# Delta-rule attention, ELU network and routed experts on one core: state products on four array quarters, a second output bank, norm steps and rounding pieces at other places

## The reference, cut to what matters

```python
# attention: 4 batches x 8 heads, 768 tokens, head size 48
k_n = k / (norm(k) + 1e-6)
for t in range(768):
    y[t] = q[t] @ state
    state += beta[t] * outer(k_n[t], v[t] - state.T @ k_n[t])
# then, on 3072 tokens of 384 features
x = elu(y @ w_in) @ w_out            # hidden 2048
logits = x @ w_gate + log1p(exp(x @ w_noise)) * noise
out = sum over the top 2 of 8 experts: weight * (relu(x @ w1[e]) @ w2[e])   # hidden 1024
```

## Time and profile before

| | us |
|---|---|
| median of three timed runs | 1183.45 (1182.54 to 1184.74) |
| the profiled execution's own time | 1186.29 |
| span of its instructions | 1184.5 |
| PE busy, share of the span | 1133.6 (96%) |
| DVE busy | 648.5 (55%) |
| ACT busy | 461.3 (39%) |
| POOL busy | 356.1 (30%) |
| mean granted TensorE clock | 0.991 |

### The profile page before, as it was taken

One profiled execution on the slowest core, in us unless ns is written; L12 is line 12 of the kernel. 1 busy time (PEld: TensorE's weight loads), 2 busy tenths in 40 slices (PEclk: granted clock), 3 DMA queues, 4 the chain that ended last, 5 costly groups with the idle time before them and its releaser, 6 DMA issues.

```text
span 1184.5 us, 29112 instructions
## 1 busy us (share of the span) xinstructions
PE 1133.6 (96%) x11596; PEld 1078.9 (91%) x11596; DVE 648.5 (55%) x1552; ACT 461.3 (39%) x1048; POOL 356.1 (30%) x378
## 2 busy tenths in 40 slices
PE   5897999898999999999999999999999999999996
PEld 3895788676999999999999999999999999999995
DVE  5888777763446556564655657522535353434442
ACT  1235556666333333333343335422424243333331
POOL 4289796244000120211202012322222222223223
PEclk9999999999999999999999999999999999999998
DMA  7453445853999110101101011472424242424221
GB/s 156 130 126 72 110 102 141 216 153 99 391 363 325 62 42 20 41 34 47 41 20 41 1 63 57 172 230 65 170 64 170 64 172 74 171 87 158 64 72 52
DMA packets 82603, 137.30 MB, mean 116 GB/s; under 512 B 11050, under 2 KB 70034, under 8 KB 81466
## 3 DMA queue, kind: packets, MB, share of 16 engines
q1 hardware_dynamic: 68490, 87.97, 25.8%
q0 software_dynamic: 12992, 28.75, 7.6%
q10 hardware_dynamic: 1008, 18.97, 4.3%
HBM read 81.96 MB, written 53.77 MB: 115 GB/s over the span
## 4 chain that ended last, share of the span: by engine, by line
PE 73%; DVE 1%; issue 0%; ACT 0%; POOL 0%; ACTq 0%; POOLq 0%
PE ps_x L1385 18%; PE ps_x L1475 18%; PE ps_h L1374 17%; PE ps_h L1453 17%; PE ps_r L1433 2%; PE ps_r L1424 1%; DVE hg L1793 0%; ACT hg L1583 0%; POOL out_dram L1340 0%; DVE w_parts L1756 0%; PE ps_r L1492 0%; DVE x_raw L1786 0%; PE ps_r L1402 0%; ACT yT_d L1601 0%; PE ps_r L1400 0%
## 5 line engine op out<-in xcount | busy, mean ns | idle before, releaser
L1475 PE MATMUL ps_x<-hg,w_parts 128*128 128x400 f32 x1152 | 230.2, 346 | 0.0
L1385 PE MATMUL ps_x<-w_parts,hg 128*128 128x400 f32 x1152 | 229.6, 345 | 0.0
L1374 PE MATMUL ps_h<-xg,w_parts 128*128 128x384 f32 x1152 | 222.3, 338 | 0.0
L1453 PE MATMUL ps_h<-xg,w_parts 128*128 128x400 f32 x1116 | 220.6, 345 | 1.1 <-DVE w_parts L1756 1.1
L1385 PEld LDWEIGHTS ps_x<-w_parts,hg 128*128 128x128 f32 x1152 | 209.7, 188 | 0.0
L1374 PEld LDWEIGHTS ps_h<-xg,w_parts 128*128 128x128 f32 x1152 | 204.0, 188 | 2.5 <-DVE elu_parts L1650 2.5
L1453 PEld LDWEIGHTS ps_h<-xg,w_parts 128*128 128x128 f32 x1116 | 202.7, 188 | 4.0 <-issue 3.1
L1475 PEld LDWEIGHTS ps_x<-hg,w_parts 128*128 128x128 f32 x1152 | 206.0, 188 | 0.0
L1793 DVE SCALAR_TENSOR_TENSOR hg<-ps_h,hg 128x400 fp32r<-128x400 f32 x128 | 73.5, 574 | 241.4 <-ACT hg L1583 238.6
L1320 POOL DMA_INDIRECT xs_scratch<-x,rows_now x48 | 49.3, 1027 | 393.5 <-DVE rows_now L1730 294.6
L1583 ACT ACTIVATE hg<-ps_h 128x400 fp32r<-128x400 f32 x128 | 64.7, 505 | 254.5 <-PE ps_h L1453 250.2
(11 more groups left out here) (175 smaller groups left out, 1325.9 us busy)
## 6 DMA issues: line engine op xcount, KB each, us to landing
xs_scratch<-pads SPq DMA_DIRECT2D x2, 5502.0 KB, 41.9
x_rows<-xs_scratch SPq DMA_DIRECT2D x17, 614.1 KB
kqT<-in_kqT_dram SPq DMA_DIRECT2D x48, 192.0 KB, 4.3
carried<-in_w_dram ACTq DMA_DIRECT2D x3, 3072.0 KB
w_raw<-in_w_dram ACTq DMA_DIRECT2D x3, 3072.0 KB
xs_scratch<-pads SPq DMA_DIRECT2D x6, 1375.5 KB, 16.8
out_dram<-pads SPq DMA_DIRECT2D x1, 4800.0 KB, 29.3
xs_scratch<-pads SPq DMA_DIRECT2D x6, 786.0 KB
```

Source lines behind the costliest of these rows:

```text
L1374: mm = nc.tensor.matmul(ps_h[f % 2][:, 0:TB], wi[:, a, k, f * P:(f + 1) * P], xr[:, b, k, :], start=(i == 0), stop=(i == len(passes) - 1))
L1385: mm = nc.tensor.matmul(ps_x[t][:, 0:DG], act_r[:, f % RING, a, t * P:(t + 1) * P], wo[:, b, f, :], start=(f == 0 and i == 0), stop=(f == ...
L1453: mm = nc.tensor.matmul(ps_h[f % 2][:, 0:TR], w1, xg[:, b, k, :], start=(m == 0), stop=(m == len(passes) - 1))
L1475: mm = nc.tensor.matmul(ps_y[k][:, 0:TR], w2r[i][:, a, s, k * P:(k + 1) * P], hg[:, s % RING, b, :], start=(s == 0 and m == 0), stop=(s == ...
```

## The change

- `ps_y` becomes two banks (4 and 5). The output of pair of heads p and half h goes to bank p % 2 and to rows `64 * (h ^ p % 2)`. The state's products contract over 48 rows (a half) in place of 128, four of them together, before the chunk's own four.
- The updates of the state, of both parities, move to bank 1, beside the keys on the state of odd chunks; `updates` gets one more wait.
- The outputs of a chunk are stored by four DMAs of half the size in place of two; the counts waited for double.
- `KEEP_BUSY` goes from 12 to 29.
- DVE: `to_set_lanes(2,(4,))` moves from ahead of the loop to the end of pair 0, (5,) and the squares to the end of pair 1; the other norm steps of group 2 move from the middle of pair 1 to pair 2, three single steps between its other work and four (`gains`) at its end. `place(1,0)` moves from the end of pair 2 into pair 3, `place(2,1)` from inside pair 7 to its end.
- ACT: the three rounding pieces of a pair move forward, to before `take_solved(a,1)`, `take_solved(b,1)` and `take_solved(a,2)`; `root_of(2)` moves to pair 2.

```diff
-KEEP_BUSY = 12
+KEEP_BUSY = 29
-        ps_y, ps_s = psum[:, 4], psum[:, 5]
+        ps_y = psum[:, 4:6, 0:2 * P].rearrange("p b (q t) -> p b q t", t=P)
+        ps_s = [psum[:, 1, i * NP * DH:(i + 1) * NP * DH] for i in range(2)]
+        def output_rows(p, h):
+            return slice(PADH * (h ^ p % 2), PADH * (h ^ p % 2) + DH)
             def store(n):
-                for h in range(2):
-                    sp.dma_start(xt_dram.rearrange("(p h d) t -> h d p t", h=2, d=DH)[h, :, :, at:at + C], yT[n % 2][heads(h)]
-                                 ).then_inc(outputs_stored[n % 2], 16)
+                for b in range(2):
+                    for h in range(2):
+                        sp.dma_start(xt_dram.rearrange("(q e d) t -> e d q t", e=4, d=DH)[2 * b + h, :, :, at:at + C],
+                                     yT[n % 2][output_rows(b, h)].rearrange("d (q b) t -> d q b t", b=2)[:, :, b]
+                                     ).then_inc(outputs_stored[n % 2], 16)
 # outputs, on PE
-                for p in range(NP):
-                    for h in range(2 if n >= B else 0):
-                        nc.tensor.matmul(ps_y[heads(h), p * P:(p + 1) * P], state[n % B][:, p, h * DH:(h + 1) * DH],
-                                         kqT[n % DEEP][:, p // QP, 1, p % QP, :], start=True, stop=False)
-                    for h in range(2):
-                        mm = nc.tensor.matmul(ps_y[heads(h), p * P:(p + 1) * P], x[n % KEPT][:, 2 * p + h, :],
+                for q in range(NP // 2):
+                    four = [(p, h) for p in (2 * q, 2 * q + 1) for h in range(2)]
+                    for p, h in four if n >= B else ():
+                        nc.tensor.matmul(ps_y[output_rows(p, h), p % 2, q], state[n % B][heads(h), p, h * DH:(h + 1) * DH],
+                                         kqT[n % DEEP][heads(h), p // QP, 1, p % QP, :], start=True, stop=False)
+                    for p, h in four:
+                        mm = nc.tensor.matmul(ps_y[output_rows(p, h), p % 2, q], x[n % KEPT][:, 2 * p + h, :],
                                               lq[n % KEPT][:, 2 * p + h, 1, :], start=(n < B), stop=True)
 # updates, on PE
+                if n >= 2:
+                    pe.wait_ge(rhs_ready[1], n // 2)
 # ACT, pair m
+                if m == 2:
+                    root_of(2)
                 if now:
+                    round_next()
                     take_solved(a, 1)
+                    round_next()
                     take_solved(b, 1)
                     round_next()
                     take_solved(a, 2)
...
-                    if m == 1:
-                        root_of(2)
-                    round_next()
                     take_solved(b, 2)
...
                     take_solved(a, 3)
-                    round_next()
 # DVE, pair m
-            to_set_lanes(2, (4,))
...
                 residuals(a, 1)
+                if m == 2:
+                    invert_root(2)
...
+                if m == 2:
+                    divide_by_root(2)
+                if m == 3:
+                    place(1, 0)
                 residuals(a, 2)
+                if m == 2:
+                    refine_root(2)
...
-                if m == 1:
-                    take_norms(2)
-                    turn_norms(2)
-                if m == 7:
-                    place(2, 1)
...
-                if m == 0:
-                    to_set_lanes(2, (5,))
+                if m < 2:
+                    to_set_lanes(2, (4 + m,))
+                if m == 1:
                     square_norms(2)
                 if m == 2:
-                    place(1, 0)
+                    gains(2)
+                    turn_norms(2)
...
-                if m == 6:
-                    place(2, 0)
+                if m in (6, 7):
+                    place(2, m - 6)
```

More of the change, by code:

```diff
@@ L364, in _ @@
                 if m == PAIRS - 2:
-                    sp.wait_ge(outputs_stored[0], (2 * B // 2 + 1) * 32)
+                    sp.wait_ge(outputs_stored[0], (2 * B // 2 + 1) * 64)
                     sp.wait_ge(vn_ready, NIT)
@@ L584, in updates @@
                         u = 2 * p + h
-                        mm = nc.tensor.matmul(ps_s[heads(h), at + p * DH:at + (p + 1) * DH], k_in[n % K_DEEP][:, u, :],
+                        mm = nc.tensor.matmul(ps_s[n % 2][heads(h), p * DH:(p + 1) * DH], k_in[n % K_DEEP][:, u, :],
                                               x[n % KEPT][:, u, :], start=True, stop=True)
@@ L710, in take_outputs @@
                 if n >= 2:
-                    act.wait_ge(outputs_stored[n % 2], n // 2 * 32)
-                nc.scalar.activation(yT[n % 2][0:PADH + DH], ps_y[0:PADH + DH].rearrange("p (a t) -> p a t", t=P), ACT.Copy
+                    act.wait_ge(outputs_stored[n % 2], n // 2 * 64)
+                nc.scalar.activation(yT[n % 2][0:PADH + DH].rearrange("p (q b) t -> p b q t", b=2), ps_y[0:PADH + DH], ACT.Copy
                                      ).then_inc(yT_ready, 1)
@@ L756, in _ @@
                     root_of(0)
-                take_blocks(i)
                 if i == 8:
                     root_of(1)
+                take_blocks(i)
                 for f in chunks_with(i):
@@ L838, in square_norms, with after_step @@
                                         ).then_inc(norm_step, 1)
[L840 to L852, removed]
-                dve.wait_ge(rooted, g + 1)
[L854 to L858, removed]
+            def after_step(g, k):
+                dve.wait_ge(norm_step, g * NORM_STEPS + k)
+                return slice(g * GSETS, (g + 1) * GSETS)
@@ new lines, in invert_root, with divide_by_root, refine_root @@
+            def invert_root(g):
+                sets = after_step(g, 1)
+                dve.wait_ge(rooted, g + 1)
+                nc.vector.reciprocal(root_inv[:, sets], root[:, sets]).then_inc(norm_step, 1)
+            def divide_by_root(g):
+                sets = after_step(g, 2)
+                nc.vector.tensor_tensor(quot[:, sets], norm2[:, sets], root_inv[:, sets], ALU.mult).then_inc(norm_step, 1)
+            def refine_root(g):
+                sets = after_step(g, 3)
+                nc.vector.tensor_tensor(root[:, sets], root[:, sets], quot[:, sets], ALU.add).then_inc(norm_step, 1)
@@ L859, in take_norms, with gains @@
+            def gains(g):
+                sets = after_step(g, 4)
+                nc.vector.tensor_scalar(norm_lane[:, sets], root[:, sets], 0.5, EPS, ALU.mult, ALU.add).then_inc(norm_step, 1)
+                after_step(g, 5)
+                nc.vector.reciprocal(root_inv[:, sets], norm_lane[:, sets]).then_inc(norm_step, 1)
                 if g == 0:
                     dve.wait_ge(beta_loaded, 16)
-                step(nc.vector.tensor_tensor(gain[:, sets], beta_sb[:, sets], root_inv[:, sets], ALU.mult))
@@ L862, in take_norms @@
-                step(nc.vector.tensor_tensor(gain[:, sets], gain[:, sets], root_inv[:, sets], ALU.mult))
+                after_step(g, 6)
+                nc.vector.tensor_tensor(gain[:, sets], beta_sb[:, sets], root_inv[:, sets], ALU.mult).then_inc(norm_step, 1)
+                after_step(g, 7)
+                nc.vector.tensor_tensor(gain[:, sets], gain[:, sets], root_inv[:, sets], ALU.mult).then_inc(norm_step, 1)
+                after_step(g, 8)
+            def take_norms(g):
+                invert_root(g)
+                divide_by_root(g)
+                refine_root(g)
+                gains(g)
@@ L915, in update_state @@
                     dve.wait_ge(ks_done[n % 2], (n - B) // 2 + 1)
-                at = n % 2 * NP * DH
                 for h in range(2):
                     s = state[n % B][heads(h), :, h * DH:(h + 1) * DH]
-                    nc.vector.tensor_tensor(s, s, ps_s[heads(h), at:at + NP * DH].rearrange("p (a d) -> p a d", d=DH), ALU.add
+                    nc.vector.tensor_tensor(s, s, ps_s[n % 2][heads(h)].rearrange("p (a d) -> p a d", d=DH), ALU.add
                                             ).then_inc(state_updated[n % 2], 1)
@@ L947, in _ @@
             dve.wait_ge(from_lanes, GSETS)
-            nc.vector.memset(ps_y, 0.0).then_inc(y_cleared, 1)
-            to_set_lanes(2, (4,))
+            nc.vector.memset(psum[:, 4:6], 0.0).then_inc(y_cleared, 1)
             for m in range(PAIRS):
@@ L1239, in _ @@
             for i in range(2):
-                sp.wait_ge(outputs_stored[i], PAIRS * 32)
+                sp.wait_ge(outputs_stored[i], PAIRS * 64)
             sp.dma_start(x_raw[:], xt_v[:, :, TB:2 * TB]).then_inc(x_loaded, 16)
@@ L1294, in _ @@
             for i in range(2):
-                pool.wait_ge(outputs_stored[i], PAIRS * 32)
+                pool.wait_ge(outputs_stored[i], PAIRS * 64)
             nc.gpsimd.memset(ones[:], 1.0).then_inc(consts_set, 1)
```

1 line of the change is left out of this document (removed).

## The result

| | before | after |
|---|---|---|
| median of the comparison, us | 1185.66 (1182.54 to 1189.29) | 1188.97 (1185.55 to 1194.5) |
| span of the profiled execution, us | 1184.5 | 1187.2 |
| mean granted clock | 0.991 | 0.991 |

The ratio is 1.003, 95% interval 1.0019 to 1.0041: slower by 3.3 us. The second part starts at 297.2 us of the span, 2.7 later than in the earlier trace rows, and takes as long as before. So, as in the prediction, everything is decided in the twelve pairs.

The account below looks back on a forecast made before the run. PE runs unbroken from 294.54 us, so only that start can move; pairs 3 to 6 are PE-bound. +2.7 (end of pair 8) - 2.1 (pairs 9 and 10) = +0.6, from the median 1183.45 giving 1184.0 us, range 1177.5 to 1189.5.

Parts of the forecast that it names:

- third rival: SP becomes the bound and the clock falls at each wait for keys in pairs 4 to 7: 1188.3 us, chance 0.16.
- Start: Loop start: first ACT copy 4.26 us earlier with fewer keep-clock matmuls, +1.8 for a cold clock in pair 0.
- Pairs 1 and 2: Together 31.6 us against 37.45, -5.8; the 4.12 us stall goes and pair 3 starts at 127.0.
- SP term: SP's queue: four more stores a pair, +2.14 us; chunk 14's keys land at 188.0, waits in pairs 4 to 6.
- POOL: Scaling of group 2 starts at 129.9, not 124.19; net for the next columns +1.6 us.
- Pair 6: Runs 2.0 us later than before; the 8.3 us earlier start of pair 3 is lost in waits for keys.
- Pair 8: Third weight piece lands at 230.6, its rounding ahead of needed copies; the pair ends at 236.9, not 234.20: +2.7.
- Pairs 9 and 10: Rounding where ACT idles frees PE: -2.1 us, bounds -4.1 and 0.
- Outputs: Each of 20 outputs on four quarters: -0.44 us from halved state groups, +0.42 from three tiling changes, net 0.0.
- The first: Rival: SP's queue keeps up and the third weight piece is in time for pair 8: 1179.4 us, chance 0.20.
- The fourth: Rival: cold start, pair 0 and part of pair 1 at the low clock level: 1188.5 us, chance 0.10.
- The second: Rival: everything arrives, POOL and SP follow the faster start, quarters' matmuls shrink: 1168 us, chance 0.08.

Follow-up runs that it names:

- run 1: Kernel before with only the short warm-up, three keep-clock matmuls of the elimination's steps instead of twenty: 1181.63 us, ratio 0.9957.
- run 3: Kernel after with SP issuing the keys that follow chunk 2m-2 ahead of the two loads of v: 1178.63 us, ratio 0.9944 to before.
- run 5: Kernel after with group 2's norms, their transposes and lane transposes back at the old places: 1183.65 us, ratio 0.9989 to before.
- run 4: Kernel after with the three roundings of a pair back at their old places: 1190.67 us, ratio 1.0045 to before.
- run 11: Kernel before with the new outputs alone (four quarters, the bank, four stores a chunk, the added wait): 1186.08 us, ratio 0.9999.
- run 2: Kernel after with the outputs as before (full 128 rows, old banks, two stores a chunk): 1181.61 us, ratio 0.9977 to before.
- run 6: Kernel before with each chunk's output stored by four half-size DMAs instead of two: 1187.05 us, ratio 1.0019.
- run 7: Kernel after with old outputs and two stores, and SP issuing keys ahead of the loads of v: 1176.54 us, ratio 0.9928 to before.

## Why the prediction was right, and where it was not

Forecast: +0.6 us over before, range 1177.5 to 1189.5. Measured: +3.3, at 1188.97, inside the range and near its upper end. It is outside the forecast's own range (1181 to 1187) and next to the third rival's 1188.3, which had a chance of 0.16; on the comparison's own before (1185.66, where the prediction had 1183.45) the sum would say 1186.3, 2.7 too low. That PE's early gain would not survive and that nothing large would come of it held. The sizes and places did not all, and errors of both signs partly cancelled, which is luck.

- *Start.* Predicted -4.26 with +1.8 for a cold clock. Pair 0 came 4.9 earlier and its first solve took 0.88 us, so in this trace the price was 0. In eight of the ten profiles with the short warm-up it was some 0.4 to 0.8 us (run 1), well under 1.8. Run 1 shows most of the gain lasting.
- *Pairs 1 and 2.* Predicted 31.6 us together, measured 36.0. Pair 1 alone (14.83) kept the promise. **The step that failed is in the SP term**: I looked for late keys "in pairs 4 to 6" and took the cost of an added issue as zero "up to pair 5", counting SP's idle time there as slack. It was not slack but a wait for POOL, with the keys behind it. With PE 11.4 us early, chunk 6's keys cost 4.87 us in pair 2, and the low clock made PE's own work there 1.9 longer (16.18, not 14.29 as in run 3, where the pair takes 16.11 in all). Pair 3 therefore started at 128.94, not 127.0; the two mistakes, of the clock and of the keys, partly cancel.
- *POOL.* Scaling of group 2 predicted at 129.9, measured 131.72 with 9.19 us idle, not some 6: pair 3 was late by the 1.9 of the step above. The mechanism is right, and run 5 shows that with the old order of SP it costs more than the stall it replaces.
- *Pair 6.* Predicted 2.0 later than before, measured 1.7 (183.96). The keys' first use is at 189.13, predicted "near 188". The way there was not 8.3 us of plain waits: 3.23 us of wait in pair 5 and the clock at 0.84 (21.43 us).
- *Pair 8.* The third piece was issued at 225.57 and landed 7.0 later, at 232.6, not 230.6; the waits for keys in pairs 7 and 8 (1.33 and 1.55) were not in the sum. The pair ended at 238.72: +4.5, not +2.7. Of the two terms of the sum this is the one further off (1.8). That the piece stands ahead of needed copies is right for pair 8 (run 4: 16.46), but moving it back gains nothing overall.
- *Pairs 9 and 10.* Predicted -2.1, measured 34.97 against 35.47, -0.5; another 1.4 came in pair 11. Measured parts: +4.5 - 0.5 - 1.4 = +2.6 in the spans (2.7). *The last store,* put at +0.3, is in that: PE's idle time before the second part grew from 0.96 to 1.36.
- *Outputs.* Predicted 0.0 for each, measured 0.0 (run 11). The Trainium skill (TensorEngine Tiling (Array Packing), Key Properties) says a change of tiling mode drains the engine. The trace agrees as far as it goes: had the halved state groups taken 2 x 0.22 = 0.44 and the own part its old 0.98, outputs would take 1.42 us and not 1.88. The 0.46 more is close to what the prediction had for three changes (0.42). That the groups were halved in time and the rest is the changes is the prediction's reading; the trace shows only their sum.
- *Rivals.* The first (the queue keeps up, 1179.4) is out, for the third piece was late. The third (waits with a falling clock, 1188.3) had the size, and its mechanism holds at two waits, of chunks 6 and 12, not at each of pairs 4 to 7. The fourth (cold start) is refuted in its size by run 1. The second (1168) shows its sense in run 3: once the keys arrive, pair 3 starts at 122.2.

How the parts add up, in per cent of the time before:

| | keys behind v | keys first |
|---|---|---|
| all of the change | +0.30 | -0.56 |
| without the new outputs | -0.23 | -0.72 |
| without the norms' placement | -0.11 | (not run) |
| without both | (not run) | -0.48 |
| start alone | -0.43 | -0.48 |

The placement of the norms costs 0.4% in the left column (+0.30 against -0.11, intervals apart) and gains 0.24 in the right one (from -0.48 to -0.72, intervals overlapping). The first figure is from kernels with the new outputs, the second from kernels with the old. With the old outputs and keys behind v, runs 2 and 1 are nearest: they differ in norms and rounding, +0.20 (intervals overlapping). The new outputs with their four stores cost 0.53 on the left (intervals apart) and 0.16 on the right (overlapping). What the parts are worth depends on one order in one queue. What stays open: whether the last 0.16 and 0.24 are real; how much of the 0.53 is the stores alone; and why run 6 and run 11, with the same stores, differ by 0.2% within overlapping intervals.

## What to carry to other kernels

Before making the bottleneck engine arrive earlier, list for each queue served in order what stands at its head and for whom: idle time there is not slack if the item that idles is waiting for a third engine and the item that you need is behind it. Issue what the bottleneck engine needs ahead of what waits for another engine. And do not judge the parts of a bundle one by one on the old order: here a removed stall was a loss until the queue was reordered, then a likely gain.

## What was unexpected of the hardware

- The clock fell behind some single waits of PE: behind 4.87 and 3.23 us of idle time the pair had PEclk 0.84 and PE was busy 1.9 and 2.5 us longer for the same work (16.18 against 14.29 in run 3; 18.06 against 15.59 in pair 6), while 3.10 us in pair 5 of run 7 and 1.99 in run 3 left it at 1.00. Length alone does not order them: after only 2.49 us in run 2 the 16 matmuls took 1.92 us, after 3.10 in run 7 they took 1.08.
- Most of the warm-up was not worth its time: with three matmuls of the steps in place of twenty the loop began 3.6 us earlier in run 1 and 4.9 in the kernel after, and the slow first solves cost at most 0.8 us of PE's time. PEclk of the stage (1.00) did not show them; their length did (1.49 us against 0.88).
- An issue on SP is not a constant: four stores took 2.01 us at 108.68 (kernel after) and 3.35 at 180.20 (run 6).
- Weight loads on quarters made PEld's busy time smaller, 11.57 us against 12.68 in a pair, and the pair's length stayed 15.66 (run 11): in the trace they overlap the matmuls.
